# Attention and two MLPs on one core: first features in halves, first keys' copy moved, weight splits released two chunks later

## What is computed

```python
f = 1 / (1 + np.exp(-f_logit))
for t in range(S):                       # per batch and head
    state = f[t, :, None] * state + outer(k[t], v[t])
    y[t] = q[t] @ state
x = y as (tokens, 384)
h = x @ moe_w_in;  x = (h * tanh(softplus(h))) @ moe_w_out            # 384 -> 2048 -> 384
x = (sigmoid(x @ w_gate) * (x @ w_val)) @ w_out                       # 384 -> 1536 -> 384
```

## Time and profile before

| what | value |
|---|---|
| median of three runs | 1002.49 us (1002.46 to 1004.06) |
| profiled execution, its own time | 1002.34 us |
| its span | 1000.2 us |
| granted TensorE clock, mean | 1.00 |
| PE busy | 986.4 us, 99% |
| DVE busy | 536.7 us, 54% |
| ACT busy | 521.7 us, 52% |
| POOL busy | 130.7 us, 13% |
| attention, from the first suffix scan to the first matmul of the first MLP | 4.45 to 147.86 us |

### The profile page before, as it was taken

One profiled execution on the slowest core, in us unless ns is written; L12 is line 12 of the kernel. 1 busy time (PEld: TensorE's weight loads), 2 busy tenths in 40 slices (PEclk: granted clock), 3 DMA queues, 4 the chain that ended last, 5 costly groups with the idle time before them and its releaser, 6 DMA issues.

```text
span 1000.2 us, 14354 instructions
## 1 busy us (share of the span) xinstructions
PE 986.4 (99%) x4925; PEld 822.7 (82%) x4925; DVE 536.7 (54%) x767; ACT 521.7 (52%) x894; POOL 130.7 (13%) x150
## 2 busy tenths in 40 slices
PE   8999999999999999999999999999999999999998
PEld 7899898888878888878888888888888888888886
DVE  8999986767767777678777322222222222222222
ACT  5666677778888888888777222221311111321122
POOL 2323326000000000045444300000000000000000
PEclk9999999999999999999999999999999999999999
DMA  7666631000000000011111100000100000100001
GB/s 243 193 202 216 196 111 56 9 1 1 1 1 0 0 0 0 0 32 47 50 49 51 34 1 1 1 1 1 64 0 0 0 0 0 64 1 0 1 1 64
DMA packets 36492, 42.27 MB, mean 42 GB/s; under 512 B 2912, under 2 KB 24928, under 8 KB 36448
## 3 DMA queue, kind: packets, MB, share of 16 engines
q1 hardware_dynamic: 36304, 41.43, 13.3%
q10 hardware_dynamic: 144, 0.26, 0.1%
HBM read 36.96 MB, written 4.72 MB: 42 GB/s over the span
## 4 chain that ended last, share of the span: by engine, by line
PE 85%; DVE 8%; issue 4%; ACT 2%; DVEq 1%; DMA 0%; ACTq 0%
PE banks L915 28%; PE banks L917 27%; PE banks L916 27%; DVE suffix L710 3%; DVE prefix L727 3%; PE banks L961 1%; PE banks L946 1%; DVE probs L744 1%; DVE sets L688 0%; DVE kb L720 0%; PE banks L966 0%; DVE state L758 0%; ACT sets L447 0%; ACT sets L440 0%; DMA xb<-f_dram 0%
## 5 line engine op out<-in xcount | busy, mean ns | idle before, releaser
L915 PE MATMUL banks<-xhi,whi 128*128 (+1 forms) x720 | 282.9, 393 | 0.0
L917 PE MATMUL banks<-xhi,wlo 128*128 (+1 forms) x720 | 281.8, 391 | 0.0
L916 PE MATMUL banks<-xlo,whi 128*128 (+1 forms) x720 | 280.6, 390 | 0.0
L915 PE MATMUL banks<-ghi,whi 128*128 128x512 f32 x504 | 199.2, 395 | 1.4 <-DVE xraw L859 1.3
L917 PE MATMUL banks<-ghi,wlo 128*128 128x512 f32 x504 | 197.8, 392 | 0.0
L916 PE MATMUL banks<-glo,whi 128*128 128x512 f32 x504 | 196.6, 390 | 0.0
L875 DVE TENSOR_TENSOR prod<-prod,banks 128x512 f32<-128x512 f32 x72 | 49.5, 688 | 236.6 <-PE banks L917 235.9
L917 PEld LDWEIGHTS banks<-xhi,wlo 128*128 128x128 f32 x720 | 135.2, 188 | 30.4
L916 PEld LDWEIGHTS banks<-xlo,whi 128*128 128x128 f32 x720 | 135.3, 188 | 29.6
L915 PEld LDWEIGHTS banks<-xhi,whi 128*128 128x128 f32 x720 | 135.2, 188 | 28.4
L605 ACT ACTIVATE ghi<-prod 128x512 fp32r<-128x512 f32 x72 | 45.5, 632 | 203.1 <-PE banks L917 124.7
(11 more groups left out here) (77 smaller groups left out, 977.3 us busy)
## 6 DMA issues: line engine op xcount, KB each, us to landing
xb<-f_dram SPq DMA_DIRECT2D x24, 256.0 KB, 3.1
kb<-k_dram SPq DMA_DIRECT2D x24, 256.0 KB, 3.4
qb<-q_dram SPq DMA_DIRECT2D x24, 256.0 KB, 3.7
raw<-w_out_dram SPq DMA_DIRECT2D x28, 192.0 KB, 2.4
vb<-v_dram SPq DMA_DIRECT2D x24, 192.0 KB, 2.4
out_dram<-rows_out SPq DMA_DIRECT2D x13, 256.0 KB, 2.2
raw<-w_in_dram SPq DMA_DIRECT2D x16, 192.0 KB, 2.7
raw<-w_gate_dram SPq DMA_DIRECT2D x12, 192.0 KB, 2.5
```

Of the source, the lines that this page charges most:

```text
L915: pe.matmul(ps, hi, xh, start=first, stop=False)
L916: pe.matmul(ps, hi, xl, start=False, stop=False)
L917: return pe.matmul(ps, lo, xh, start=False, stop=last)
```

## The change

Three edits of the attention part:

1. The features of chunk 0 come in two transfers of two pairs each, the upper pairs first. ACT gates each half when it has landed, and DVE scans each half (the scan runs backward, so the upper one first).
2. `k_rows(0)`, ACT's copy of chunk 0's transposed keys, moves from before the gates of chunk 2 to behind the query halves of chunk 1.
3. POOL splits unit u two steps later, and each step first waits until DVE has multiplied that step's queries: unit u waits for `qdec_done` to reach u + 3, which is chunk u+2's product.

```diff
             def load_x(g, n):
+                if isinstance(g, int) and g == 0:
+                    sp.dma_start(xb[:, 0, PAIRS // 2:PAIRS], rows_of(f[0])[:, PAIRS // 2:PAIRS]).then_inc(x_upper_in, 16)
+                    sp.dma_start(xb[:, 0, 0:PAIRS // 2], rows_of(f[0])[:, 0:PAIRS // 2]).then_inc(x_in[0], 16)
+                    return
                 sp.dma_start(xb[:, n % 2], rows_of(f[g])).then_inc(x_in[n % 2], 16)
...
-            def split_unit(b, n):
-
+            def split_unit(q, i):
+
+                wait(pool, qdec_done, q * NCH + i + 1 if not isinstance(q, int) else min(q * NCH + i + 1, B * NCH))
+                if (at := lag_a(q, i, 2)) is None:
+                    return
+                b, n = at
                 unit, s = b * NCH + n, n % STAGES
...
-            run_a(pool, 0, 0, split_unit)
+            run_a(pool, 2, 2, split_unit)
...
             def gates(b, n):
 
                 g = b * NCH + n
+                if isinstance(b, int) and (b, n) == (0, 0):
+                    act.wait_ge(x_upper_in, 16)
+                    act.activation(gate_rows[:, PAIRS // 2:PAIRS, 1:C + 1], xb[:, 0, PAIRS // 2:PAIRS], ACT.Sigmoid).then_inc(upper_gate_done, 1)
+                    act.wait_ge(x_in[0], 16)
+                    act.activation(gate_rows[:, 0:PAIRS // 2, 1:C + 1], xb[:, 0, 0:PAIRS // 2], ACT.Sigmoid).then_inc(gates_done, 1)
+                    return
...
+                    if do is k_rows and isinstance(b, int) and (b, n) == (0, 1):
+                        continue
                     if at := lag_a(b, n, lag):
                         do(*at)
+                    if do is q_halves and isinstance(b, int) and (b, n) == (0, 2):
+                        k_rows(0, 0)
...
             def suffixes(b, n):
 
                 g = b * NCH + n
+                if isinstance(b, int) and (b, n) == (0, 0):
+                    half = PAIRS // 2 * (C + 1)
+                    dve.wait_ge(upper_gate_done, 1)
+                    dve.tensor_tensor_scan(flat(suffix)[:, half:2 * half][:, ::-1], gate[:, half + 1:2 * half + 1][:, ::-1],
+                                           flat(last)[:, half:2 * half][:, ::-1], 0.0, ALU.mult, ALU.add).then_inc(upper_suffix_done, 1)
+                    dve.wait_ge(gates_done, 1)
+                    dve.wait_ge(upper_suffix_done, 1)
+                    dve.tensor_tensor_scan(flat(suffix)[:, 0:half][:, ::-1], gate[:, 1:half + 1][:, ::-1],
+                                           flat(last)[:, 0:half][:, ::-1], 0.0, ALU.mult, ALU.add).then_inc(suffix_done, 1)
+                    return
```

More of the change, by code:

```diff
@@ L191, in attention_mlp_mlp @@
         x_in = [sem(f"x_in{i}") for i in range(2)]
+        x_upper_in, upper_gate_done, upper_suffix_done = sem("x_upper_in"), sem("upper_gate_done"), sem("upper_suffix_done")
         k_in = [sem(f"k_in{i}") for i in range(3)]
```

## The result

The changed kernel takes 1009.94 us (median, 1009.87 to 1010.13) against 1002.70 (1002.46 to 1004.06) of the kernel before in the same runs: ratio 1.0071, 95% interval 1.0060 to 1.0083, so 7.2 us slower where 4.5 were forecast. Its profiled execution took 1009.95 us with a span of 1008.2; the span before was 1000.2.

The account below looks back on a forecast made before the run. Attention was taken as bound by DVE until 124.4 us, then closely by PE. Splits +5.3, start -0.3 and keys' copy -0.07, less PE's lag of 0.41, gave +4.5 us: 1007.0 us, range 1003.5 to 1010.

Parts of the forecast that it names:

- What bounds attention: Attention before the first MLP matmul: bound by DVE until 124.4 us, then closely by PE until 147.86 us.
- PE's lag: End of attention: PE trails DVE by only 0.41 us; DVE losses beyond that count fully toward the end time.
- The sign that PE would wait for the halves: Attention in the new profile: PE should wait for ACT's query halves in nearly every chunk, the last ones too.
- The splits: POOL's weight splits beside DVE's suffix scans: 21 scans lose 0.52 us each, 10.9 added, 5.6 removed, net +5.3 us.
- The row behind the 0.52: Earlier trace of attention: cast began at 87.82 after the product ended at 87.79; the scan took 1.74 against 1.22 us.
- the bound of 0.70: Upper bound on a split's cost at the suffix scan, POOL starting 0.2 us later: 0.70 us each, 14.7 in all.
- The removed part: Old splits' cost to DVE's scans and products in attention: 6.0 us, of which 5.6 was to go.
- The start: Chunk 0's features in halves: upper half lands 0.35 us sooner, reciprocal at 5.38 us; gain taken as 0.3 us.
- The first keys' copy: ACT's moved copy of chunk 0's keys: DVE gains at most 0.07 us, at the suffix scan after chunk 2's gates.
- Staging and the prefetch: Weight loads on SP: later splits use staging slack without a wait; the rival of staging run dry, 1016 us, had 0.07.
- The no-change rival: Attention: a split costs 0.24 to 0.35 us, net 0 to 2.3 us on DVE, time 1002 to 1004.3; chance 0.13.
- The tail: After the last queries: units 21 to 23 split beside the first MLP input's low parts, 0 us taken, at most +1.

## Why the prediction was right, and where it was short

**What bounds attention: right.** The last queries came 7.6 us later and the first MLP matmul 7.2; the difference is PE's lag, which was used up first. The sign that PE would wait for the halves in nearly every chunk, the last ones too, did not come: it waited in 15 of 24, and the scores of the last three chunks (137.31, 143.37 and 149.50 us) started without a wait, 1.46 to 1.53 us behind their queries' product, where the last that had waited started 1.37 behind. DVE and PE are nearly level there.

**The splits: right mechanism, one term too small.** The 21 scans lost 13.9 us against 10.9 forecast. The row behind the 0.52 was a cast released by a transfer, which began 0.03 us behind the product by chance. Released by the queries inside the loop, the cast begins 0.16 to 0.27 behind it, and in three chunks the gap before the subtraction is 0.24 too, so that 18 scans lost 12.5 us, 0.69 each. The three in peeled steps lost 0.47 each. The prediction set a longer wake-up of POOL off against a shorter gap in the last units; the gap was shorter in 3 steps, the wake-up longer in 18. With the loop written out the sum is 21 x 0.47 = 9.9 and the time 1005.8. That the changed kernel's 1009.94 lies in the range at all, 0.06 us below its end, is luck in part: the 0.66 a split that came is close to the bound of 0.70, which the prediction had for just this cause, a POOL slower to start, and called hardly likely when it cut the range to 1010. The removed part, 5.6 us, was right: of the 6.0 us lost before, 0.4 stays on the products (2.6 us there became 0.4), as much as was left out by choice.

**The start: 0.5 in place of 0.3.** The upper half landed at 0.82 + 2.26 = 3.08, 0.53 sooner than the whole had, where 0.35 was assumed. The fit that the prediction cites, by which half the bytes save 0.3, is stated in the Trainium skill (DMA: Bandwidth & Descriptors, "Anatomy of one DMA") for transfers that GpSimd issues; SP issues these. The halves of 0.42 on ACT and 0.70 on DVE were as estimated. The lower half cost nothing more, since it had landed while ACT gated the upper one. The first keys' copy gave what was said, nothing to measure.

**Staging and the prefetch: right.** DVE shows no idle time before scans or products that came with the change.

**The no-change rival: priced wrongly.** At 0.24 to 0.35 us a split, 21 splits less the 5.6 give -0.6 to +1.8 us, not 0 to 2.3, and a time of 1001.1 to 1003.5. The release one instruction earlier is a case of it: 0.32 each, and 1002.97 us.

**The tail: 0 taken, 0.8 came, within the 1 allowed.** In the changed kernel the three low parts beside the last splits took 3.15 us together, against 1.90 before. No matmul waited for them. What was not foreseen is that the state products stand behind them on DVE, so that PE waited 0.39 us for a transpose behind those (L1035). It came 7.8 us later than before, and the matmuls from 172 us on 8.0.

Sum by the runs, on the last queries: 13.9 - 5.6 - 0.5 - 0.07 = +7.7, against 7.6 seen; less the lag of 0.4, 7.2 on the first matmul, and with the tail's 0.8 the 8.0 of the span. The time grew by 7.6 in the profiled executions and by 7.2 between the medians, since 2.14 us of it lay outside the span before and 1.75 now; no run tells why. That the 7.2 of the medians equals the 7.2 of the matmul is chance.

## What to carry to other kernels

When two engines contend, ask for each of their instructions what it lies beside, and lay the contending work beside the one that doesn't mind: here 1.0 us of subtraction fits behind the 1.13 us mask, and 1.7 us of cast and subtraction doesn't. A release pins work to one place in the period, for good or ill; a cost that had struck by chance in some chunks then strikes in all. Take the length from a start that was released the same way, since 0.17 us of later start, counted 18 times, makes 3 us and was most of the error here.

## What the runs showed of the hardware

POOL's start behind a DVE semaphore was 0.16 to 0.27 us in a loop over batches and 0.07 us in steps written out; the gap between its two dependent instructions went from 0.16 or 0.24 to 0.07 to 0.09.

A POOL instruction that only writes ran beside a two-input DVE scan without cost to either (0.42 and 1.22 us).

TensorE's granted clock fell once in the changed kernel while PE was waiting more. The stretches of 54 to 58 us, with columns as in the earlier trace rows:

```profile
54.00:56.00 2.00, 1.43 (x24) 1.26 (x23) 2.00 (x3) 1.85 (x4) 0.93 (x2) 1.00 0.64 229
56.00:58.00 2.00, 2.00 (x6) 1.58 (x7) 1.97 (x3) 0.99 (x3) 0.57 (x1) 0.56 0.69 191
```

A share of 0.56 is near the lower of the two levels, 1.2 GHz of 2.4. PE had waited 1.02 us at 50.30 and 0.57 at 55.95 for the query halves; the scores at 55.95 then took 3.52 us in place of 1.99. The same two waits before the scores at 125.72 and 131.37 went by at a clock of 1.00, so the waits alone don't decide it. DVE's pitch from that chunk to the next was 6.13 us, as in the same place of the next batch, so it cost nothing here.
